# Experts of a mixture of experts: transposes in two groups among the products, and the weights' high parts on GpSimd

## The chip, the cores and the metric

The kernel runs on one core of one Trainium2 chip. The metric is the device time of one execution in microseconds. TensorE does the matrix products; VectorE, ScalarE and GpSimd work element by element; SyncE issues most of the transfers. The engines run their own instruction streams and meet only at semaphores.

## The reference

```python
def reference(q, k, v, proj, moe..., moe2...):
    x = attention(q, k, v, proj)            # 2 batches, 8 heads, 768 tokens, 64 wide: 1536 tokens x 512
    x = moe(x, ...)                         # what the change is about
    return mlp(x, w_in, w_out)              # 512 -> 2048 -> 512 with softplus

def moe(x, modality_id, w_gate, modality_bias, w1, w2):      # N 1536, D 512, E 8, F 1024
    logits = x @ w_gate + modality_bias[modality_id]
    e_idx = argmax(logits, axis=1)
    gate_w = softmax(logits)[arange(N), e_idx]
    for e in range(E):
        mask = e_idx == e
        h = maximum(x[mask] @ w1[e], 0.0)
        out[mask] = gate_w[mask, None] * (h @ w2[e])
    return out
```

Everything is in float32. Each token goes to one expert.

## The kernel before

It has three stages: attention, experts, and the last two layers (here MLP). Only the experts' stage is changed.

Tokens are sorted by expert on the chip, and each expert's tokens are worked through in tiles of 128. The number of tiles of an expert is data: every engine reads it from a table and runs one loop per expert, `Fori(0, n_e)`. `g` numbers the tiles through all experts. Tile 0 (part of the favourite expert) and tile 1 are done ahead by other code; the loops do tiles 2 on.

To keep float32 exactness on TensorE's faster fp32r path, each operand is split into a high part (the value rounded to fp32r) and a low part (value minus high part), and a product is made as high x high, low x high and high x low. So for each expert:

- SyncE loads `w1s[e % 2]` and `w2s[e % 2]` (2 MB each), once the expert that used the buffers is done.
- The high parts `w1h` (in two halves of 128x2048) and `w2h` (in four quarters of 128x1024) are copies by ScalarE (`w1_high`, `w2_high`). There is one `w1h` and one `w2h`, so the copy for expert e waits for `hB_done` (the last first-layer product of the expert before), or `y_done` (its last second-layer product).
- The low parts `w1l`, `w2l` are written in place of the loaded weights by VectorE (`w1_low`, `w2_low`, lines 1187 and 1194): loaded weight minus high part, both in SBUF.

And for each tile `g`, on TensorE, in this order:

- `w1_products`: 24 products of 512 columns into `psA[1]`, first half of the hidden features (12), then the second (12); each half in three parts of four: (`xth`, `w1h`), (`xtl`, `w1h`), (`xth`, `w1l`). They signal `hA_done` and `hB_done`.
- The rows of the hidden layer are copied by ScalarE from PSUM to `hrow` (`take_rows`), and TensorE transposes them: `turn_h(g, 0)`, `turn_y(g - 1)` (the previous tile's output rows) and `turn_h(g, 1)`, four 128x128 transposes each.
- ScalarE makes `hTh` from the transposed halves (`take_h`, with the Relu), and VectorE `hTl` (`low_h`, one input in PSUM, one in SBUF).
- `w2_products`: 24 products into `ps7`: for each half, eight with `hTh` (times `w2h`, `w2l`), then four with `hTl`. The last signals `y_done`.

Beside it ScalarE and VectorE make the next tile's `xth` (`high_x`) and `xtl` (`low_x`, both inputs in SBUF), and `x2h`, `x2l` for the MLP from the transposed output (`high_x2`, `low_x2`, PSUM and SBUF). Each engine works in program order: on VectorE `w1_low(e)` and `w2_low(e)` (six instructions) stand ahead of the loop over the expert's tiles, so ahead of its first `low_h`; before the loop of the last expert stand two `split_wi` as well. GpSimd's program goes from the gathering of the tokens' rows (line 595) to the MLP's `softplus`.

Of the kernel before, what the change touches and what calls it, by code (L numbers as in the profile page):

```python
# [10 lines left out]
ACT = mybir.ActivationFunctionType  # L11
# [17 lines left out]
DC = DM // P  # L29
E, F = 8, 1024  # L30
# [9 lines left out]
RING = 2  # L40
QUART = FC // 4
# [13 lines left out]
def build(nc, qk, v, proj, modality_id, fold_gate, modality_bias, w1, w2, w_in, w_out, out):  # L55
    ctx = ExitStack()
    with ctx:
# [249 lines left out]
        def loaded(e):  # L307

            return 16 * (e // RING + 1 + e % RING)
# [132 lines left out]
        def _(pool):  # L442
# [151 lines left out]
            for n in range(TILES):  # L594
                pool.indirect_dma_start(xin[:, n, :, :].rearrange("p h e -> p (h e)"), None, x_rows[:, :],
                                        bass.IndirectOffsetOnAxis(source[:, n:n + 1], 0)).then_inc(gathered[n], 16)

            def softplus(k, u):

                wait_reg(u_done, k + 1)  # L600
                pool.tensor_tensor(hres[u][:, :], hexp[u][:, :], hres[u][:, :], ALU.subtract).then_inc(c_done, 1)  # L601
                wait_reg(sum_done, k + 1)
                wait_reg(c_done, k + 1)
                pool.tensor_tensor(hsum[u][:, :], hsum[u][:, :], hres[u][:, :], ALU.add).then_inc(s_done, 1)  # L604
# [30 lines left out]
        def _(act):  # L635
# [85 lines left out]
            act.wait_ge(xT0_done, 1)  # L721
            nc.scalar.activation(xT0[:, :, :], psA[0][:, 1, :].rearrange("p (c n) -> p c n", c=DC), ACT.Copy).then_inc(xT0_ready, 1)

            def w1_high(e, first):

                act.wait_ge(w1_in[e % RING], loaded(e))
                if e:
                    act.wait_ge(hB_done, first)
                for h in range(2):
                    fs = slice(h * F // 2, (h + 1) * F // 2)  # L730
                    nc.scalar.activation(w1h[:, :, fs], w1s[e % RING][:, :, fs], ACT.Copy).then_inc(w1h_ready, 1)

            def w2_high(e, first):

                act.wait_ge(w2_in[e % RING], loaded(e))
                if e:
                    act.wait_ge(y_done, first)
                for h in range(4):
                    fs = slice(h * QUART, (h + 1) * QUART)
                    nc.scalar.activation(w2h[:, fs, :], w2s[e % RING][:, fs, :], ACT.Copy).then_inc(w2h_ready, 1)  # L740

            def gated(n):

# [6 lines left out]
            def high_x(g, at):  # L750

                act.wait_ge(hB_done, g)
                nc.scalar.activation(xth[:, :, :], xT[:, :, bass.ds(at, P)], ACT.Copy).then_inc(xh_ready, 1)

            def take_rows(g):

                for half, done, turned, ready in ((0, hA_done, tA_done, rA_ready), (1, hB_done, tB_done, rB_ready)):
                    act.wait_ge(done, g + 1)
                    act.wait_ge(turned, g - 1)
                    nc.scalar.activation(hrow[:, half * F // 2:(half + 1) * F // 2], psA[1][:, half, :], ACT.Copy).then_inc(ready, 1)  # L760

            def take_h(g, ps, doneA, doneB, count, halves=(0, 1)):

                for half in halves:
                    done, ready = ((doneA, hAh_ready), (doneB, hBh_ready))[half]
                    act.wait_ge(done, count)
                    nc.scalar.activation(hTh[:, half * FC // 2:(half + 1) * FC // 2, :],  # L767
                                         ps[:, half, :].rearrange("p (c n) -> p c n", c=FC // 2),
                                         ACT.Relu).then_inc(ready, 1)
# [25 lines left out]
                                     ACT.Copy).then_inc(woh_ready, 1)  # L795

            act.wait_ge(x_ready, PAIRS)
            w2_high(0, 0)
            act.wait_ge(lg_ready, 1)
            nc.scalar.activation(tmp8[:, :, :], tmp8[:, :, :], ACT.Exp).then_inc(gexp_done, 1)  # L800

# [4 lines left out]
                                     psA[1][:, half, :].rearrange("p (c n) -> p c n", c=FC // 2), ACT.Relu).then_inc(hT0_ready, 1)  # L806

            take_h0(0, hA_done)
            w1_high(0, 0)
            take_h0(1, hB_done)  # L810
            act.wait_ge(table_ready, 1)
            tiles_of = experts(act)
# [22 lines left out]
            high_x(2, nc.scalar.snap(nxt, min_val=0, max_val=B * S))  # L835
            for e in range(E):
                n_e, base_e, upto_e, first = next(tiles_of) if e else of_first
                if e:
                    w1_high(e, first)
                    w2_high(e, first)  # L840
                if e == E - 1:
                    for k in range(LAG):
                        split_wi(k, k)
                with nc.scalar.Fori(0 if e else 1, n_e) as i:
                    g = first + i
                    take_y(g - 1)
                    take_rows(g)
                    take_h(g, psA[2], tA_done, tB_done, g)
                    high_x2(g - 1, nc.scalar.snap(col, min_val=0, max_val=B * S))
                    act.reg_mov(col, nxt)  # L850
                    act.reg_mov(nxt, base_e + i * P + P)
                    act.reg_alu(nxt, nxt, upto_e, ALU.min)
                    high_x(g + 1, nc.scalar.snap(nxt, min_val=0, max_val=B * S))


            def softplus(k, u):
# [68 lines left out]
        def _(dve):  # L925
# [272 lines left out]
                dve.wait_ge(xT_done, n + 1)  # L1198
                V.tensor_copy(xT[:, :, n * P:(n + 1) * P], turn[n % 2].rearrange("p (c n) -> p c n", c=DC)).then_inc(xT_ready, 1)

            def low_h(g, ps):

                for half, high, ready in ((0, hAh_ready, hA_ready), (1, hBh_ready, hB_ready)):
                    fs = slice(half * FC // 2, (half + 1) * FC // 2)
                    dve.wait_ge(high, g)
                    V.scalar_tensor_tensor(hTl[:, fs, :], ps[:, half, :].rearrange("p (c n) -> p c n", c=FC // 2),  # L1206
                                           0.0, hTh[:, fs, :].bitcast(F32), ALU.max, ALU.subtract).then_inc(ready, 1)

            def low_x(g, at):

                dve.wait_ge(xh_ready, g - 1)
                V.tensor_tensor(xtl[:, :, :], xT[:, :, bass.ds(at, P)], xth[:, :, :].bitcast(F32), ALU.subtract).then_inc(xl_ready, 1)
# [42 lines left out]
            for e in range(E):  # L1255
                n_e, base_e, upto_e, first = next(tiles_of) if e else of_first
                if e:
                    w1_low(e)
                    w2_low(e)
                if e == E - 1:  # L1260
                    for k in range(LAG):
                        split_wi(k, k)
                with nc.vector.Fori(0 if e else 1, n_e) as i:
                    g = first + i
                    low_h(g, psA[2])
                    low_x2(g - 1, nc.vector.snap(col, min_val=0, max_val=B * S))
                    dve.reg_mov(col, nxt)
                    dve.reg_mov(nxt, base_e + i * P + P)
                    dve.reg_alu(nxt, nxt, upto_e, ALU.min)
                    low_x(g + 1, nc.vector.snap(nxt, min_val=0, max_val=B * S))  # L1270

            def softplus(k, u):
                dve.wait_ge(e_done, k + 1)
# [68 lines left out]
        def _(pe):  # L1342
            T = nc.tensor
# [203 lines left out]
                    last = turned(turn[n % 2][:, c * P:(c + 1) * P], xs_bits[n % 2][:, c * P:(c + 1) * P])  # L1547
                last.then_inc(xT_done, 1)

            def w1_products(e, g):  # L1550

                pe.wait_ge(xl_ready, g - 1)
                for half, done in ((0, hA_done), (1, hB_done)):
                    pe.wait_ge(w1h_ready, 2 * e + half + 1)
                    fs = slice(half * F // 2, (half + 1) * F // 2)
                    first = True
                    for x, w in ((xth, w1h), (xtl, w1h), (xth, w1l[e % RING])):
                        if w is not w1h:
                            pe.wait_ge(w1_split, 2 * e + half + 1)
                        for c in range(DC):  # L1560
                            last = T.matmul(psA[1][:, half, :], x[:, c, :], w[:, c, fs], start=first, stop=(w is not w1h and c == DC - 1))
                            first = False
                    last.then_inc(done, 1)

            def turn_h(g, half):

# [3 lines left out]
                    last = turned(psA[2][:, half, f * P:(f + 1) * P], hrow_bits[:, at:at + P])  # L1570
                last.then_inc((tA_done, tB_done)[half], 1)

            def w2_products(e, g):

                for half, high, low in ((0, hAh_ready, hA_ready), (1, hBh_ready, hB_ready)):
                    fs = range(half * FC // 2, (half + 1) * FC // 2)
                    pe.wait_ge(high, g)
                    for f in fs:
                        if f % QUART == 0:
                            pe.wait_ge(w2_split, 4 * e + f // QUART + 1)  # L1580
                        T.matmul(ps7[:, :], hTh[:, f, :], w2h[:, f, :], start=(f == 0), stop=False)  # L1581
                        T.matmul(ps7[:, :], hTh[:, f, :], w2l[e % RING][:, f, :], start=False, stop=False)
                    pe.wait_ge(low, g)
                    for f in fs:
                        last = T.matmul(ps7[:, :], hTl[:, f, :], w2h[:, f, :], start=False, stop=(f == FC - 1))
                last.then_inc(y_done, 1)
# [27 lines left out]
            for e in range(E):  # L1614
                n_e, _, _, first = next(tiles_of) if e else of_first
                with nc.tensor.Fori(0 if e else 1, n_e) as i:
                    g = first + i
                    w1_products(e, g)
                    turn_h(g, 0)
                    turn_y(g - 1)  # L1620
                    turn_h(g, 1)
                    w2_products(e, g)
            final = next(tiles_of)[3] - 1


# [117 lines left out]
```

## Time and profile before

| | us |
|---|---|
| median of 3 runs | 745.8 (745.42 to 746.28) |
| the profiled execution | 744.41 |
| its span in the trace | 742.6 |
| TensorE at work in the span | 719.3 (97%) |
| VectorE | 570.9 (77%) |
| ScalarE | 500.1 (67%) |
| GpSimd | 318.7 (43%) |

The experts' loops run from about 284 to 470 us of the span. In the profile PE is TensorE's products (PEld its weight loads, which overlap them), DVE VectorE, ACT ScalarE, POOL GpSimd, SP SyncE; a busy time is the time in which the engine had an instruction at work. Products are pipelined: one of 512 columns is shown with 0.39 us, but the next begins 0.2265 us after it.

### The profile page before, as it was taken

To read this page: it belongs to the slowest core of one execution; us is meant where nothing else is said; L and a number is where in the kernel's file an instruction comes from. 1 tells how busy PE (TensorE), PEld (TensorE's weight loads), DVE (VectorE), ACT (ScalarE), POOL (GpSimd) and SP (SyncE) were. 2 spreads that over 40 slices of the span, in tenths; PEclk is the share of its full clock that TensorE was granted. 3 is DMA by queue.
4 is the path that set the end of the run, shared out by engine and by line. 5 is a ranking of instruction groups with operands and counts; after the bars stand their busy time and mean duration, and the time that the engine had idled before them with its cause. 6 is when DMAs were issued, how large, how long until landed. Compare 5 with 4: busy or idle time off the path is not lost. (4 is left out here: it accounts for less than half of the span.)

```text
span 742.6 us, 13137 instructions
## 1 busy us (share of the span) xinstructions
PE 719.3 (97%) x4017; PEld 607.1 (82%) x4017; DVE 570.9 (77%) x944; ACT 500.1 (67%) x916; POOL 318.7 (43%) x289
## 2 busy tenths in 40 slices
PE   5999999999999999999999999999999999999996
PEld 4888888989988778888888878778887888878884
DVE  6999999999999666449992181598788787887874
ACT  6888788888887654559993372565656656566562
POOL 7777566778741450000000000155554755557543
PEclk9999999999999999999999999999999999999999
DMA  3811111104133268328991000032322423225221
GB/s 128 291 49 44 53 38 46 59 18 161 40 109 137 100 195 333 117 113 315 353 357 51 0 29 0 30 113 85 113 86 85 167 87 110 90 86 169 85 85 57
DMA packets 40531, 85.05 MB, mean 115 GB/s; under 512 B 5584, under 2 KB 9840, under 8 KB 40496
## 3 DMA queue, kind: packets, MB, share of 16 engines
q1 hardware_dynamic: 37776, 77.01, 30.4%
q0 software_dynamic: 2000, 6.98, 2.8%
q10 hardware_dynamic: 720, 0.64, 0.2%
q8 instruction: 17, 0.28, 0.2%
q14 instruction: 18, 0.15, 0.1%
HBM read 76.82 MB, written 6.68 MB: 112 GB/s over the span
## 5 line engine op out<-in xcount | busy, mean ns | idle before, releaser
L601 POOL TENSOR_TENSOR hres<-hexp,hres 128x512 f32<-128x512 f32 x46 | 59.7, 1298 | 303.7 <-DVE hres L1274 303.6
L668 ACT ACTIVATE pTh<-psA 128x384 fp32r<-128x384 f32 x192 | 83.9, 491 | 38.2 <-PE psA L1382 37.8
L949 DVE TENSOR_TENSOR pTl<-psA,pTh 128x384 fp32r<-128x384 f32 x192 | 97.7, 551 | 8.8 <-ACT pTh L668 7.9
L1376 PE MATMUL psA<-K,Q 128*128 128x384 f32 x384 | 92.5, 364 | 3.3 <-ACT K L705 2.1
L942 DVE TENSOR_SCALAR_CACHE_REDUCE psA<-psA 128x768 f32<-128x768 f32 x96 | 91.8, 956 | 3.2 <-PE psA L1376 3.1
L659 ACT ACTIVATE probs<-psA,negmax 128x768 f32<-128x768 f32 x96 | 87.4, 910 | 2.9 <-DVE psA L942 2.5
L1222 DVE TENSOR_TENSOR wil<-rawi,wih 128x512 fp32r<-128x512 f32 x48 | 79.1, 1650 | 6.6 <-ACT wih L787 6.6
L859 ACT ACTIVATE habs<-psA 128x512 f32<-128x512 f32 x48 | 28.6, 597 | 76.8 <-PE psA L1638 76.8
L1206 DVE SCALAR_TENSOR_TENSOR hTl<-psA,hTh 128x512 fp32r<-128x512 f32 x32 | 21.4, 688 | 73.1 <-ACT hTh L767 72.8
L1382 PEld LDWEIGHTS psA<-ident_r,probs_bits 128*128 128x128 f32 x576 | 59.3, 143 | 17.3 <-issue 6.8
L604 POOL TENSOR_TENSOR hsum<-hsum,hres 128x512 f32<-128x512 f32 x46 | 69.6, 1514 | 8.2 <-POOL hres L601 8.2
L1652 PE MATMUL psA<-woh,sh 128*128 128x512 f32 x184 | 72.1, 392 | 0.7 <-DVE sl L1291 0.7
L1382 PE MATMUL psA<-ident_r,probs_bits 128*128 128x128 f32 x576 | 70.8, 252 | 1.3 <-DVE pTl L949 0.7
L1653 PE MATMUL psA<-wol,sh 128*128 128x512 f32 x184 | 71.6, 389 | 0.0
L1654 PE MATMUL psA<-woh,sl 128*128 128x512 f32 x184 | 71.6, 389 | 0.0
L1376 PEld LDWEIGHTS psA<-K,Q 128*128 128x128 f32 x384 | 64.2, 193 | 6.1 <-issue 4.9
L1405 PE MATMUL ps<-pTh,vhl 128*128 128x384 f32 x186 | 62.8, 338 | 0.1
L1405 PE MATMUL ps<-pTl,vhl 128*128 128x384 f32 x186 | 62.5, 336 | 0.0
L1291 DVE TENSOR_TENSOR sl<-hsum,sh 128x512 fp32r<-128x512 f32 x47 | 53.6, 1140 | 1.8 <-ACT sh L873 1.8
L1638 PE MATMUL psA<-x2h,wih 128*128 128x512 f32 x192 | 51.7, 391 | 0.8 <-DVE hsum L1282 0.7
L1581 PE MATMUL ps<-w2h,hTh 128*128 128x512 f32 x128 | 51.6, 403 | 0.0
L1638 PE MATMUL psA<-x2l,wih 128*128 128x512 f32 x192 | 51.4, 389 | 0.0
(243 smaller groups left out, 1656.1 us busy)
## 6 DMA issues: line engine op xcount, KB each, us to landing
w2s<-in_moe_w SPq DMA_DIRECT2D x9, 2048.0 KB, 9.4
w1s<-in_moe_w SPq DMA_DIRECT2D x9, 2048.0 KB, 9.1
rawi<-in_moe_w_in SPq DMA_DIRECT2D x48, 256.0 KB, 2.6
rawo<-in_moe_w_out SPq DMA_DIRECT2D x48, 256.0 KB, 2.8
raw<-in_qk SPq DMA_DIRECT2D x16, 384.0 KB, 3.1
vs<-in_v SPq DMA_DIRECT2D x16, 192.0 KB, 2.4
x_rows<-X SPq DMA_DIRECT2D x1, 1728.0 KB, 6.8
x_rows<-X SPq DMA_DIRECT2D x1, 1512.0 KB, 5.5
```

The lines of the kernel that those rows point to most:

```text
L659: nc.scalar.activation(probs[u % 2][:, :].rearrange("p (a n) -> p a n", a=2), psA[u % 2][:, :, 0:HALF], ACT.Exp, bias=negmax[:, u % 4:u % ...
L668: nc.scalar.activation(pTh[u // TPGR % 2][:, g * TPH:(g + 1) * TPH, u % TPGR * P:(u % TPGR + 1) * P], psA[2][:, g, 0:HALF].rearrange("p (t ...
L942: V.tensor_scalar(psA[u % 2][:, :, 0:HALF], psA[u % 2][:, :, 0:HALF], PENALTY, PENALTY, ALU.min, ALU.min, accum_out=negmax[:, u % 4:u % 4 ...
L949: V.tensor_tensor(pTl[u // TPGR % 2][:, g * TPH:(g + 1) * TPH, cols], psA[2][:, g, 0:HALF].rearrange("p (t n) -> p t n", t=TPH), pTh[u // ...
L1222: V.tensor_tensor(wil[u][:, :, :], rawi[u][:, :, :], wih[u][:, :, :].bitcast(F32), ALU.subtract).then_inc(wi_split, 1)
L1376: last = T.matmul(psA[u % 2][:, h, 0:HALF], qs[par][:, cols], ks[par][:, h * HALF:(h + 1) * HALF], start=start, stop=not start)
L1382: return T.transpose(out.bitcast(F32R), rows_bits, ident_r[:, :])
L1405: last = T.matmul(last_ps if type(G) is int and G == PAIRS - 1 else ps6[:, 0:COLS], vhl[gm // 2 % 2][:, kt, :], p[gm % 2][:, kt, :], start ...
L1638: last = T.matmul(hps[u], w[u][:, d, :], x[:, d, g * GTOK:(g + 1) * GTOK], start=first, stop=(w is wil and d == DC - 1))
L1652: T.matmul(acc[t], sh[u][:, cols], woh[u][:, :], start=first, stop=False)
L1653: T.matmul(acc[t], sh[u][:, cols], wol[u][:, :], start=False, stop=False)
L1654: last = T.matmul(acc[t], sl[u][:, cols], woh[u][:, :], start=False, stop=final)
```

## The change

On TensorE the two groups of transposes of hidden rows are moved apart. The tile's order becomes: the twelve products of the first half; parts 0 and 1 of the second half; `turn_h(g, 0)` and `turn_y(g - 1)`; part 2 of the second half; the eight high products of the first half of the second layer; `turn_h(g, 1)`; the rest. ScalarE and VectorE order their per-half work to match. And for experts 1 to 7 the copies that make `w1h` and `w2h` go from ScalarE to GpSimd, which in this stage had nothing to do; expert 0's stay on ScalarE. `wait_reg` is GpSimd's wait on a semaphore followed by an increment of another.

```diff
+            pool.wait_ge(table_ready, 1)
+            tiles_of = experts(pool)
+            next(tiles_of)
+            for e in range(1, E):
+                _, _, _, first = next(tiles_of)
+                wait_reg(w1_in[e % RING], loaded(e))
+                wait_reg(hB_done, first)
+                for h in range(2):
+                    fs = slice(h * F // 2, (h + 1) * F // 2)
+                    pool.tensor_copy(w1h[:, :, fs], w1s[e % RING][:, :, fs]).then_inc(w1h_ready, 1)
+                    wait_reg(w1h_ready, 2 * e + h + 1)
+                wait_reg(w2_in[e % RING], loaded(e))
+                wait_reg(y_done, first)
+                for h in range(4):
+                    fs = slice(h * QUART, (h + 1) * QUART)
+                    pool.tensor_copy(w2h[:, fs, :], w2s[e % RING][:, fs, :]).then_inc(w2h_ready, 1)
+                    wait_reg(w2h_ready, 4 * e + h + 1)
...
             for e in range(E):
                 n_e, base_e, upto_e, first = next(tiles_of) if e else of_first
-                if e:
-                    w1_high(e, first)
-                    w2_high(e, first)
...
                 with nc.scalar.Fori(0 if e else 1, n_e) as i:
                     g = first + i
                     take_y(g - 1)
-                    take_rows(g)
-                    take_h(g, psA[2], tA_done, tB_done, g)
+                    take_rows(g, 0)
+                    take_h(g, psA[2], tA_done, tB_done, g, (0,))
                     high_x2(g - 1, nc.scalar.snap(col, min_val=0, max_val=B * S))
...
+                    take_rows(g, 1)
                     high_x(g + 1, nc.scalar.snap(nxt, min_val=0, max_val=B * S))
+                    take_h(g, psA[2], tA_done, tB_done, g, (1,))
...
-                    low_h(g, psA[2])
+                    low_h(g, psA[2], (0,))
                     low_x2(g - 1, nc.vector.snap(col, min_val=0, max_val=B * S))
...
                     low_x(g + 1, nc.vector.snap(nxt, min_val=0, max_val=B * S))
+                    low_h(g, psA[2], (1,))
...
+            def w1_products(e, g, half, parts):
+
+                done = (hA_done, hB_done)[half]
+                fs = slice(half * F // 2, (half + 1) * F // 2)
+                for part in parts:
+                    x, w = ((xth, w1h), (xtl, w1h), (xth, w1l[e % RING]))[part]
...
@@ w2_products
                         T.matmul(ps7[:, :], hTh[:, f, :], w2l[e % RING][:, f, :], start=False, stop=False)
+                    if half == 0 and turning:
+                        turn_h(g, 1)
                     pe.wait_ge(low, g)
...
                     g = first + i
-                    w1_products(e, g)
+                    pe.wait_ge(xl_ready, g - 1)
+                    w1_products(e, g, 0, (0, 1, 2))
+                    w1_products(e, g, 1, (0, 1))
                     turn_h(g, 0)
                     turn_y(g - 1)
-                    turn_h(g, 1)
-                    w2_products(e, g)
+                    w1_products(e, g, 1, (2,))
+                    w2_products(e, g, turning=True)
```

## Rows read from the trace of the kernel before

**Rows 1.** Windows of two tiles: us, busy of PE, PEld, DVE, ACT, POOL, PEclk, DMA, GB/s

```profile
309.00:321.40 12.40, 12.35 (x62) 10.16 (x61) 2.59 (x4) 3.90 (x7) 0.00 (x0) 1.00 0.00 0
...
370.86:383.21 12.35, 12.29 (x61) 10.12 (x60) 11.44 (x11) 11.18 (x13) 0.00 (x0) 1.00 0.91 336
```

**Rows 2.** Timeline of ScalarE, experts' stage: start us, us, what

```profile
296.98 3.91 ACT L740 ACTIVATE w2h<-w2s 128x1024 fp32r<-128x1024 f32 x4 [0.52 <-PE ps L1585]
...
329.80 3.72 ACT L731 ACTIVATE w1h<-w1s 128x2048 fp32r<-128x2048 f32 x2
334.05 3.91 ACT L740 ACTIVATE w2h<-w2s 128x1024 fp32r<-128x1024 f32 x4 [0.54 <-PE ps L1585]
...
383.47 3.91 ACT L740 ACTIVATE w2h<-w2s 128x1024 fp32r<-128x1024 f32 x4 [0.52 <-PE ps L1585]
...
432.91 3.91 ACT L740 ACTIVATE w2h<-w2s 128x1024 fp32r<-128x1024 f32 x4 [0.53 <-PE ps L1585]
```

**Rows 3.** Waits of 285 to 472 us: total us, times, longest

```profile
PEld psA L1382 <- ACT hrow L760: 3.8, 15, 1.0
```

**Rows 4.** Timeline of one tile's turn from first to second layer

```profile
375.40 1.07 PE L1561 MATMUL psA<-w1l,xth 128*128 128x512 f32 x4
...
376.31 0.45 PE L1382 MATMUL psA<-ident_r,hrow_bits 128*128 128x128 f32 x4
...
376.51 0.60 ACT L760 ACTIVATE hrow<-psA 128x512 f32<-128x512 f32 x1 [0.51 <-PE psA L1561]
...
377.16 0.40 PEld L1382 LDWEIGHTS psA<-ident_r,hrow_bits 128*128 128x128 f32 x4 [0.20 <-ACT hrow L760]
...
377.65 0.50 PE L1581 MATMUL ps<-w2h,hTh 128*128 128x512 f32 x1
```

**Rows 5.** Timeline of TensorE where the MLP begins

```profile
471.28 1.07 PE L1638 MATMUL psA<-x2l,wih 128*128 128x512 f32 x4
472.19 1.07 PE L1638 MATMUL psA<-x2h,wil 128*128 128x512 f32 x4
473.10 0.46 PE L1382 MATMUL ps<-ident_r,yrow_bits 128*128 128x128 f32 x4
...
474.40 1.08 PE L1638 MATMUL psA<-x2l,wih 128*128 128x512 f32 x4
```

**Rows 6.** GpSimd's casts, groups by form: busy us, mean ns, idle before

```profile
L515 POOL CAST vhl<-vs 128x384 fp32r<-128x384 f32 x16 | 8.0, 503 | 50.0 <-PE ps L1405 50.0
...
L464 POOL CAST ident_r<-ident 128x128 fp32r<-128x128 f32 x1 | 0.3, 288 | 0.0
```

**Rows 7.** Timeline of VectorE, boundary to expert 7

```profile
429.01 0.68 DVE L1212 TENSOR_TENSOR xtl<-xT,xth 128x512 fp32r<-128x512 f32 x1
430.61 4.50 DVE L1187 TENSOR_TENSOR w1l<-w1s,w1h 128x2048 fp32r<-128x2048 f32 x2 [0.92 <-ACT w1h L731]
435.02 4.62 DVE L1194 TENSOR_TENSOR w2l<-w2s,w2h 128x1024 fp32r<-128x1024 f32 x4
...
439.56 1.29 DVE L1222 TENSOR_TENSOR wil<-rawi,wih 128x512 fp32r<-128x512 f32 x2
```

**Rows 8.** Timeline of GpSimd and VectorE, three places where they meet

```profile
500.72 1.52 POOL L604 TENSOR_TENSOR hsum<-hsum,hres 128x512 f32<-128x512 f32 x1 [0.18 <-POOL hres L601]
501.01 1.78 DVE L1222 TENSOR_TENSOR wil<-rawi,wih 128x512 fp32r<-128x512 f32 x1
...
212.17 0.83 POOL L497 CAST Q<-qs 64x768 fp32r<-64x768 f32 x1
...
212.55 0.48 DVE L1032 TENSOR_SCALAR chosen<-chosen,code 128x8 f32<-128x8 f32 x1
...
6.62 0.95 DVE L1099 TENSOR_TENSOR K<-raw,K 64x768 fp32r<-64x768 f32 x1
6.87 0.91 POOL L488 CAST K<-bits 12x192 fp32r<-12x192 f32 x1 [0.44 <-DVE bits L1097]
```

**Rows 9.** VectorE's PSUM-reading subtraction: duration ns min/median/max, first, last start

```profile
L949 DVE TENSOR_TENSOR pTl<-psA,pTh x192: 540/548/560, 15.5 to 243.8; 128x384 fp32r<-128x384 f32 x192
```

**Rows 10.** Granted clock in 40 slices, and TensorE's longest wait (total, times, longest)

```profile
PEclk9999999999999999999999999999999999999999
...
PE ps L1353 <- ACT hashc L695: 4.5, 1, 4.5
```

More of the change, by code:

```diff
@@ L722, in _, with w1_high_first, w2_high_first @@
             nc.scalar.activation(xT0[:, :, :], psA[0][:, 1, :].rearrange("p (c n) -> p c n", c=DC), ACT.Copy).then_inc(xT0_ready, 1)
-            def w1_high(e, first):
-                act.wait_ge(w1_in[e % RING], loaded(e))
-                if e:
-                    act.wait_ge(hB_done, first)
+            def w1_high_first():
+                act.wait_ge(w1_in[0], loaded(0))
                 for h in range(2):
                     fs = slice(h * F // 2, (h + 1) * F // 2)
[L731 to L737, printed above, removed]
+                    nc.scalar.activation(w1h[:, :, fs], w1s[0][:, :, fs], ACT.Copy).then_inc(w1h_ready, 1)
+            def w2_high_first():
+                act.wait_ge(w2_in[0], loaded(0))
                 for h in range(4):
                     fs = slice(h * QUART, (h + 1) * QUART)
-                    nc.scalar.activation(w2h[:, fs, :], w2s[e % RING][:, fs, :], ACT.Copy).then_inc(w2h_ready, 1)
+                    nc.scalar.activation(w2h[:, fs, :], w2s[0][:, fs, :], ACT.Copy).then_inc(w2h_ready, 1)
             def gated(n):
@@ L753, in high_x, with take_rows @@
                 nc.scalar.activation(xth[:, :, :], xT[:, :, bass.ds(at, P)], ACT.Copy).then_inc(xh_ready, 1)
[L755 to L760, printed above, removed]
+            def take_rows(g, half):
+                done, turned, ready = ((hA_done, tA_done, rA_ready), (hB_done, tB_done, rB_ready))[half]
+                act.wait_ge(done, g + 1)
+                act.wait_ge(turned, g - 1)
+                nc.scalar.activation(hrow[:, half * F // 2:(half + 1) * F // 2], psA[1][:, half, :], ACT.Copy).then_inc(ready, 1)
             def take_h(g, ps, doneA, doneB, count, halves=(0, 1)):
@@ L797, in _ @@
             act.wait_ge(x_ready, PAIRS)
-            w2_high(0, 0)
+            w2_high_first()
             act.wait_ge(lg_ready, 1)
@@ L808, in _ @@
             take_h0(0, hA_done)
-            w1_high(0, 0)
+            w1_high_first()
             take_h0(1, hB_done)
@@ L837, in _ @@
                 n_e, base_e, upto_e, first = next(tiles_of) if e else of_first
-                if e:
-                    w1_high(e, first)
-                    w2_high(e, first)
                 if e == E - 1:
@@ L1199, in take_xT, with low_h @@
                 V.tensor_copy(xT[:, :, n * P:(n + 1) * P], turn[n % 2].rearrange("p (c n) -> p c n", c=DC)).then_inc(xT_ready, 1)
-            def low_h(g, ps):
-                for half, high, ready in ((0, hAh_ready, hA_ready), (1, hBh_ready, hB_ready)):
+            def low_h(g, ps, halves=(0, 1)):
+                for half in halves:
+                    high, ready = ((hAh_ready, hA_ready), (hBh_ready, hB_ready))[half]
                     fs = slice(half * FC // 2, (half + 1) * FC // 2)
@@ L1548, in turn_x @@
                 last.then_inc(xT_done, 1)
[L1550 to L1563, printed above, removed]
+            def w1_products(e, g, half, parts):
[3 more added lines that the diff above has]
+                    x, w = ((xth, w1h), (xtl, w1h), (xth, w1l[e % RING]))[part]
+                    if part == 0:
+                        pe.wait_ge(w1h_ready, 2 * e + half + 1)
+                    elif part == 2:
+                        pe.wait_ge(w1_split, 2 * e + half + 1)
+                    for c in range(DC):
+                        last = T.matmul(psA[1][:, half, :], x[:, c, :], w[:, c, fs], start=(part == 0 and c == 0),
+                                        stop=(part == 2 and c == DC - 1))
+                    if part == 2:
+                        last.then_inc(done, 1)
             def turn_h(g, half):
@@ L1571, in turn_h, with w2_products @@
                 last.then_inc((tA_done, tB_done)[half], 1)
-            def w2_products(e, g):
+            def w2_products(e, g, turning=False):
                 for half, high, low in ((0, hAh_ready, hA_ready), (1, hBh_ready, hB_ready)):
```

## The prediction

> **What bounds the kernel now.** I read the windows of single tiles first. In the experts' stage a tile of 128 tokens takes 12.35 to 12.4 us with TensorE at work for all but some 0.05 us of it, whether it is a middle tile of a long expert (VectorE at work 2.59 us) or a one-tile expert (VectorE 11.44, ScalarE 11.18, GpSimd 0.00) [rows 1]. So TensorE sets the pace of all 15 looped tiles, but in one-tile experts VectorE and ScalarE have under 1 us of slack each. The starts of w2's high parts on ScalarE give the layout: expert 0 ends at 296.98; 37.07 us (three tiles) later expert 1 ends at 334.05; from there to 383.47 four boundaries lie 12.35 us apart, so experts 2 to 5 have one tile each; expert 6 has four tiles (to 432.91) and expert 7 the last three [rows 2]. GpSimd does nothing in the stage.
>
> Then the waits. In the stage TensorE's weight loads wait for ScalarE's copy of the second half of the hidden rows: 3.8 us in 15 waits, 0.25 a tile [rows 3]. In the timeline of one tile the twelve transposes begin at 376.31, are held 0.20 us before the last four until the copy that started at 376.51 ends, and the second-layer products begin at 377.65 [rows 4].
>
> **What the change saves.** 48 products 512 wide at 0.2265 us (0.907 for four, from 471.28 to 472.19 and on) are 10.87 us; the tile's other 1.48 us are the twelve transposes with their wait and switches. Four transposes alone between products, nothing waited for, cost this: from 472.19 to 474.40 are eight products (1.81) and one such group, 0.40 us [rows 5]. Three fours are 1.2 us. With the third part of the second half's products and then the high products of the first half between copy and transpose, neither copy is waited for: 0.28 us less a tile, 12.07 us, for 15 tiles -4.2 us. Lower bound of the gain: 0, if the extra switch between transposes and products eats it; no row shows the new order. take_rows, take_h, low_h are only reordered; their 0.6 and 0.69 us stay off the path, since first-half rows still have products and transposes between them and their use.
>
> **What GpSimd's copies cost alone.** For each of experts 1 to 7, two copies of 128x2048 and four of 128x1024. GpSimd's casts take 0.288 us for 128 elements and 0.503 for 384, so 0.18 + 0.00084 n: 1.89 us and 1.04 us [rows 6]. That is what ScalarE takes (3.72 for two, 3.91 for four [rows 2]), 8 us of GpSimd in a 12.35 us tile. Taken alone it fits, and ScalarE is relieved of 7.6 us an expert; but ScalarE wasn't on the path, so this relief earns nothing beyond the 4.2.
>
> **What they cost together with VectorE.** The low parts are VectorE subtractions with both inputs in SBUF: two in 4.50 us, four in 4.62, and low_x 0.68 [rows 7]. The trace shows what happens when GpSimd works in SBUF at the same time. VectorE's 128x512 subtraction, 0.68 us alone [rows 7], took 1.78 from 501.01, to 502.79: 0.55 after GpSimd's instruction ended at 502.24. An instruction of only 8 elements a partition took 0.48 and ended at 213.03, with GpSimd's cast of 212.17 ending at 213.00. The other way, a cast of only 12x192 took 0.91 us and ended at 7.78, 0.21 after VectorE's two-input subtraction ended at 7.57 [rows 8]. So whoever comes second waits for the whole instruction, and that holds for casts too. Where VectorE reads one input from PSUM nothing is lost: 192 such subtractions beside GpSimd's work stay between 540 and 560 ns [rows 9]; hTl and x2l are of that kind.
>
> The Trainium skill ("SBUF — State Buffer", Who interferes with whom) says the same as a rule: a VectorE instruction with two SBUF inputs and a GpSimd one that reads SBUF share a port pair under an exclusive lock, and the second to issue fully blocks. By it no part of a copy would overlap a subtraction, as in my sum; the rows above agree for instructions under 1.8 us, and no row shows 2 us casts. Without it (rows for short ones not carrying over) the sum would be -4.2 alone.
>
> Pure passes, start-up excluded (GpSimd 0.836 n ns; VectorE n/0.96 ns, of whose 0.68 us for 512 that leaves 0.15 of start-up): copies 2x1.71 + 4x0.86 = 6.8; subtractions 2x2.13 + 4x1.07 + 0.53 = 9.1; together 15.9 us of the shared resource per expert. With every start-up counted it is 17.7. A one-tile expert offers 12.07.
>
> **The queue at a boundary**, 0 being hB_done of the previous expert's last tile. GpSimd wakes at some 0.18 (its gap at 500.72 [rows 8]): first half of w1h to 2.1; low_x behind it to 2.6; second half to 4.3; hTl's second half (needs no port) 3.7; w1l first to 6.4; then alternately (y_done is at 5.8, so GpSimd now queues too) w2h quarter 0 to 7.3, w1l second 9.4, quarter 1 10.3, w2l 0 11.4, quarter 2 12.2, w2l 1 13.3, quarter 3 14.1, w2l 2 15.2, w2l 3 16.3, and only then, VectorE being in order, hTl's first half of the new tile, 17.0. TensorE begins the new tile at 5.7, finds both halves of w1 in time (needed at 5.7 and 8.4; low ones 7.5 and 11.0), reaches the second layer at 11.9, waits 0.6 for w2l 1, transposes to 14.6 and waits 2.4 for hTl. Loss: 3.0 us, at experts 1 and 6. At experts 2 to 5 the next expert's w1 copy (its hB_done was at 11.9) is already queued behind quarter 3 and gets in ahead of w2l 3: 1.7 more, 4.7; the tile is 16.8, not far over the 15.9 of passes. At expert 7 VectorE has two w_in splits as well before hTl (1.29 us for two [rows 7]): 4.2.
>
> Sum: 4x4.7 + 2x3.0 + 4.2 = 29.0, less 4.2: **+24.8 us**. Profiled execution 744.4 (its span 742.6 and 1.8 around): 769.2. The median of the runs, 745.8, is 1.4 above that execution: 770.6, forecast **770.5**.
>
> Bounds. Below: only part of each copy excludes VectorE, half the loss: 29.0/2 - 4.2 = +10, 756. Above: every hand-over is paid in full with start-up and semaphore: two times (1.89 + 0.18 + 2.28 + 0.05), four times (1.04 + 0.18 + 1.22 + 0.05), low_x 0.68 (0.05 as from ScalarE's end at 377.11 to 377.16 [rows 4]): 19.4 us, so +7.4 over 12.07 four times; at the other boundaries some 1.5 of the 2.6 that this adds to 16.8 lies ahead of hTl, so 4.5 twice and 5.7 once; less 4.2: +40, 786. I take the alternation since the rows show a blocked instruction ending 0.55 after its release, a pass without start-up.
>
> **Rivals.**
> 1. Faster: the exclusion doesn't carry over to long casts (or is brief at their start), so the copies hide in idle GpSimd. Place: w1l and w2l; price 0; it decides if copy and subtraction overlap so far that the per-expert chain is under 12.07 us instead of 15.9. Then -4.2: 741.6. For it: GpSimd idle all stage, ScalarE near full. Against: three kinds of collisions in the trace. 5 in 100.
> 2. Half the loss, 756, by partial overlap or a luckier order of grants. 11 in 100.
> 3. Paid in full, 786: VectorE or GpSimd keeps coming too late for a grant. 10 in 100.
> 4. TensorE's clock falls in the new stalls of about 4 us. In every slice it is granted in full now, and the longest wait, 4.5 us, stands ahead of the first products [rows 10], so the trace says neither. Price: the 16 products left of the second layer (3.6 us) at 1.2 instead of 2.4 GHz take 3.6 more, at five boundaries up to 18: 788. 9 in 100. The Trainium skill ("TensorE: Matmul & The Clock Gate", summary table) advises against idle gaps between bursts for this reason; no run here shows it.
> 5. The change doesn't do what it says in its order part: transposes still wait, gain 0, 774. Within the forecast's range.
>
> The forecast with 5 has 65 in 100; likely range 764 to 776. The range for 8 in 10 reaches from 2 to 3: 756 to 786. About 0.2% (1.5 us) is what can be told from no change. Faster 0.06 (rival 1 and a bit of 2), same 0.02, slower 0.92.
>
> **What would show it.** VectorE's w1l subtractions up from 2.28 us to about 4 and w2l from 1.22 to about 2 where casts run; GpSimd casts also lengthened above 1.89 and 1.04; a wait of TensorE for hTl at each boundary's first low products, 2.4 us at experts 1 and 6 and 4 at 2 to 5; tiles without a boundary at 12.07 with no wait for hrow. Wrong if casts and subtractions keep their lengths side by side, if the tile of experts 2 to 5 stays near 12.1, or if the granted clock falls below full after the stalls.

## The result

Before 745.51 us (six runs, 744.98 to 746.28), after 776.24 us (six runs, 775.08 to 779.65): ratio 1.0411, 95% interval 1.0397 to 1.0426, 30.7 us slower. The forecast was 770.5, range 756 to 786. The profiled execution of the changed kernel has a span of 773.3 us against 742.6, 30.7 more.

All but 0.4 us of it lies in the experts' loops. In the changed kernel the first copy of output rows after tile 1 starts at 284.99 and the last at 501.28, 216.3 us for 15 tiles; between the same copies of the kernel before it is 186.0 (284.56 to 470.58, ScalarE's line 774). The page of the kernel after: share of busy time of each engine, then of the 40 slices the rows of TensorE and of its clock.

```profile
PE 728.8 (94%) x4017; PEld 612.7 (79%) x4017; DVE 600.9 (78%) x944; ACT 450.5 (58%) x874; POOL 405.4 (52%) x331
...
PE   5999999999999998997798997999999999999996
...
PEclk9999999999999999998999999999999999999998
```

Windows of single tiles, which answer to [rows 1]: first tile of expert 1, a middle tile of it, then experts 2, 3, 4 and 5 (one tile each), first tiles of 6 and 7. Columns as there; the last but two is the granted clock.

```profile
296.81:313.71 16.90, 14.04 (x61) 11.12 (x60) 13.34 (x10) 4.00 (x7) 7.90 (x4) 0.90 0.43 154
313.71:325.78 12.07, 12.07 (x62) 9.96 (x60) 2.69 (x4) 4.00 (x7) 0.00 (x0) 1.00 0.00 0
337.82:357.16 19.34, 14.82 (x61) 11.67 (x60) 19.34 (x12) 4.00 (x7) 12.88 (x6) 0.82 0.66 241
357.16:370.79 13.63, 12.24 (x61) 10.05 (x60) 9.89 (x10) 4.01 (x7) 11.79 (x6) 1.00 0.84 309
370.79:391.20 20.41, 15.32 (x61) 11.63 (x60) 20.41 (x12) 4.00 (x7) 13.86 (x6) 0.83 0.56 207
391.20:404.74 13.54, 12.25 (x61) 10.05 (x60) 9.80 (x10) 4.01 (x7) 11.69 (x6) 1.00 0.90 329
404.74:422.66 17.92, 14.52 (x61) 10.99 (x60) 14.29 (x10) 4.00 (x7) 8.84 (x4) 0.90 0.45 162
458.84:476.96 18.12, 14.10 (x61) 11.10 (x60) 14.52 (x12) 4.00 (x7) 7.87 (x4) 0.91 0.09 29
```

The middle tile takes 12.07 us as forecast, ScalarE is at work for 4 us in any tile, and the seven first tiles of experts 1 to 7 take 119.9 us where the kernel before needed 87.2 (six of 12.34 to 12.38, and 13.01 at expert 7, where TensorE waited 0.62 us for hrow). VectorE is at work without a gap in experts 2 and 4, and in three of the rows shown the clock's mean is 0.90 or 0.91, in two 0.82 and 0.83. (The kernel before had 1.00 in both [rows 1].)

The waits of TensorE in the stage (total, times, longest; PE's rows, as the wait of the weight load before it repeats the same time) show who held it:

```profile
PE ps L1603 <- DVE hTl L1220: 18.4, 7, 3.9
...
PE ps L1597 <- DVE w2l L1207: 4.2, 7, 0.7
```

The wait for hrow of [rows 3] is gone. The groups of casts and subtractions in the stage (busy us, mean ns | idle before):

```profile
L613 POOL CAST w2h<-w2s 128x1024 fp32r<-128x1024 f32 x28 | 55.5, 1982 | 20.6 <-PE ps L1603 17.1 <-POOL w2h L613 3.5
...
L1207 DVE TENSOR_TENSOR w2l<-w2s,w2h 128x1024 fp32r<-128x1024 f32 x28 | 48.9, 1788 | 7.5 <-POOL w2h L613 7.5
L1200 DVE TENSOR_TENSOR w1l<-w1s,w1h 128x2048 fp32r<-128x2048 f32 x16 | 44.7, 2834 | 0.0
...
L607 POOL CAST w1h<-w1s 128x2048 fp32r<-128x2048 f32 x14 | 31.5, 2248 | 85.5 <-PE psA L1576 82.4 <-POOL w2h L613 1.9 <-POOL w1h L607 1.2
```

Alone a cast of 1024 takes 1.05 us and one of 2048 1.90 (their shortest in this trace, at 391.54 and 332.29); the means are 1.98 and 2.25. The w2l subtraction goes from 1.22 us (mean in the kernel before; four in 4.62 in [rows 7]) to 1.79, the w1l subtraction from 2.29 to 2.83.

And this is what follows the waits. Timeline of TensorE, the first four products with hTl after each wait, experts 1 to 4:

```profile
308.40 2.08 PE L1603 MATMUL ps<-w2h,hTl 128*128 128x512 f32 x4 [2.22 <-DVE hTl L1220]
...
351.09 2.08 PE L1603 MATMUL ps<-w2h,hTl 128*128 128x512 f32 x4 [3.92 <-DVE hTl L1220]
...
367.03 1.20 PE L1603 MATMUL ps<-w2h,hTl 128*128 128x512 f32 x4 [1.39 <-DVE hTl L1220]
...
385.04 2.08 PE L1603 MATMUL ps<-w2h,hTl 128*128 128x512 f32 x4 [3.92 <-DVE hTl L1220]
```

Four such products take 1.07 us at the full clock. After the waits shown of 2.22 and 3.92 us they take 2.08, the lower level, 1.2 GHz: in the window 308.40 to 311.80 the granted clock is 0.52, in 351.00 to 354.50 it is 0.50. The moment of the fall differs: at expert 2 it lies within the wait (1.00 until 349.20, 0.52 in the next us, the wait ends at 351.09), at expert 7 only after the wait of 3.42 us (1.00 until 472.00, the wait ended at 471.61, 0.56 in the next us). After the wait of 1.39 us they take 1.20, as after any restart. From the end of the wait to the next tile's first product there are 16 products: 3.76 us at expert 3, but 5.31, 6.07, 6.16, 5.37 and 5.35 us at experts 1, 2, 4, 6 and 7 (waits of 2.22, 3.92, 3.92, 2.22 and 3.42 us). The sum over 3.76 is **9.5 us** that the lower clock costs.

### The profile page after: what moved, and what is told of

Same layout as the page of the kernel before. It is cut to its first block and busy times, and to the rows that moved or that the text cites. A ratio compares the mean times of both kernels' runs of the same rounds, so it can differ in the third digit from the quotient of the medians.

```text
span 773.3 us, 13225 instructions
## 1 busy us (share of the span) xinstructions
PE 728.8 (94%) x4017; PEld 612.7 (79%) x4017; DVE 600.9 (78%) x944; ACT 450.5 (58%) x874; POOL 405.4 (52%) x331
## 5 line engine op out<-in xcount | busy, mean ns | idle before, releaser
L607 POOL CAST w1h<-w1s 128x2048 fp32r<-128x2048 f32 x14 | 31.5, 2248 | 85.5 <-PE psA L1576 82.4
L613 POOL CAST w2h<-w2s 128x1024 fp32r<-128x1024 f32 x28 | 55.5, 1982 | 20.6 <-PE ps L1603 17.1
L1207 DVE TENSOR_TENSOR w2l<-w2s,w2h 128x1024 fp32r<-128x1024 f32 x32 | 53.7, 1717 | 7.5 <-POOL w2h L613 7.5
L1597 PE MATMUL ps<-w2h,hTh 128*128 128x512 f32 x128 | 54.6, 427 | 4.2 <-DVE w2l L1207 4.2
```

## The experiments

The experiments ran on two chips on which the kernel before takes 752.7 and 752.6 us instead of 745.5; so ratios and differences to it are compared.

**The order alone.** GpSimd's block is left out, and ScalarE has the copies again:

```diff
                 n_e, base_e, upto_e, first = next(tiles_of) if e else of_first
+                if e:
+                    w1_high(e, first)
+                    w2_high(e, first)
```

> The new order of products and transposes alone; all high parts stay on ScalarE. Account of the prediction (ScalarE is not on the path, the order gains 0.28 us in each of 15 tiles): 745.5 - 4.2 = 741.3 us. Rival: on ScalarE the second half of hTh now comes after the second layer has begun, so at a boundary the six copies of weights start later and end later, and the copy of the next tile's first rows, queued behind them, is late for transposes that the new order wants eight products earlier: about 1.2 us of wait for hrow at each of 7 boundaries, the tiles without a boundary still at 12.06. That gives 745.5 + 7 x 0.9 - 8 x 0.29 = about 749.5 us.

Measured: ratio 1.0039 (1.0025 to 1.0052), 2.8 us slower (755.49 against 752.69). The rival was right, in kind and in size (4 us were expected). Timeline of the first tile of expert 1:

```profile
305.85 3.89 ACT L740 ACTIVATE w2h<-w2s 128x1024 fp32r<-128x1024 f32 x4
...
309.64 0.58 ACT L774 ACTIVATE yrow<-ps 128x512 f32<-128x512 f32 x1
310.12 0.59 ACT L760 ACTIVATE hrow<-psA 128x512 f32<-128x512 f32 x1
310.76 0.54 PE L1386 MATMUL psA<-ident_r,hrow_bits 128*128 128x128 f32 x4 [0.77 <-ACT hrow L760]
```

TensorE waits 0.77 us for rows that ScalarE copies only after the four quarters of w2h, and the boundary tiles of experts 1 to 6 take 13.07 us, that of expert 7, after a wait of 1.82, 14.10; tiles without a boundary take 12.05. So the order's gain of 0.28 us a tile is real in eight tiles and is lost in seven. In the changed kernel it is had everywhere only because ScalarE has been relieved.

**GpSimd's copies alone.** The kernel before, with the new block on GpSimd and without `w1_high`, `w2_high` in the loop on ScalarE:

```diff
                 n_e, base_e, upto_e, first = next(tiles_of) if e else of_first
-                if e:
-                    w1_high(e, first)
-                    w2_high(e, first)
```

> The old order of products and transposes, with the high parts of experts 1 to 7 on GpSimd. If the loss is the collision of casts and subtractions alone, it is all here, plus the 4.2 us that the order gives back: 745.5 + 30.7 + 4 = about 780 us, and tiles without a boundary stay at 12.35. If the new order has a part in the loss (the second half of hTl, made late, stands ahead of w1's low parts on VectorE), it is clearly less: 770 us or under.

Measured: 1.0424 (1.0405 to 1.0444), 31.0 us slower (783.66). The loss is here without the new order. 35 were expected, the 30.7 and the order's gain. The tiles without a boundary are at 12.36 to 12.40, so they lose some 2.5 us against the changed kernel; but the seven first tiles take 117.3 us, 2.6 less than there. In them TensorE waits 0.4 us for w2l instead of 4.2, and about as long for hTl:

```profile
PE ps L1600 <- DVE hTl L1221: 19.4, 7, 4.2
```

The clock falls at four of the seven boundaries here, not at five. Experts 1 and 2 wait nearly the same time, and only at expert 2 does the clock fall (timeline of TensorE):

```profile
314.94 1.21 PE L1600 MATMUL ps<-w2h,hTl 128*128 128x512 f32 x4 [2.75 <-DVE hTl L1221]
...
355.09 2.07 PE L1600 MATMUL ps<-w2h,hTl 128*128 128x512 f32 x4 [2.69 <-DVE hTl L1221]
```

The granted clock is 1.00 from 312.10 to 318.94, through the first wait and all products after it, and 0.50 from 355.09 to 358.00.

**GpSimd writes, but doesn't read.**

```diff
-                    pool.tensor_copy(w1h[:, :, fs], w1s[e % RING][:, :, fs]).then_inc(w1h_ready, 1)
+                    pool.memset(w1h[:, :, fs].bitcast(F32), 0.0).then_inc(w1h_ready, 1)
...
-                    pool.tensor_copy(w2h[:, fs, :], w2s[e % RING][:, fs, :]).then_inc(w2h_ready, 1)
+                    pool.memset(w2h[:, fs, :].bitcast(F32), 0.0).then_inc(w2h_ready, 1)
```

> As the changed kernel, but GpSimd fills w1h and w2h with zeros instead of copying the weights into them (so the products with the high parts of experts 1 to 7 are left out of the result): as many elements written, nothing read from SBUF. If the loss comes of GpSimd and VectorE both reading SBUF, it goes away and only the gain of the order is left: 741.3 us, subtractions back at 2.28 and 1.22 us, every tile at 12.06. If GpSimd's mere activity or its place in the chain of semaphores is the cause, it stays within 10 us of 776.

Measured: 0.9947 (0.9933 to 0.9960), 3.8 us faster (748.89 against 752.69). Groups by form in the stage:

```profile
L1200 DVE TENSOR_TENSOR w1l<-w1s,w1h 128x2048 fp32r<-128x2048 f32 x16 | 35.9, 2282 | 0.0
...
L613 POOL MEMSET w2h<- 128x1024 f32 x28 | 26.8, 958 | 17.9 <-PE ps L1603 14.7 <-POOL w2h L613 3.2
L607 POOL MEMSET w1h<- 128x2048 f32 x14 | 25.4, 1815 | 97.4 <-PE psA L1576 96.3 <-POOL w1h L607 1.1
```

Fills nearly as long as the casts alone, in the same chain of semaphores, and the subtractions are back at 2.28 us; the tiles of the stage, boundaries too, take 12.06 us but for expert 7's first, 12.38. So neither GpSimd's activity nor its place in the chain costs anything: what costs is that it reads SBUF. That VectorE must read it with both inputs shows in the changed kernel, where three VectorE instructions of 512 columns, 0.68 us each when alone, fall beside one cast (timelines of GpSimd and VectorE):

```profile
349.52 2.66 POOL L607 CAST w1h<-w1s 128x2048 fp32r<-128x2048 f32 x1 [0.17 <-POOL w1h L607]
...
350.35 0.68 DVE L1220 SCALAR_TENSOR_TENSOR hTl<-psA,hTh 128x512 fp32r<-128x512 f32 x1
350.95 0.68 DVE L1231 TENSOR_TENSOR x2l<-ps,x2h 128x512 f32 x1
351.55 1.17 DVE L1226 TENSOR_TENSOR xtl<-xT,xth 128x512 fp32r<-128x512 f32 x1
```

The two with an input in PSUM keep their 0.68 us; the one with both inputs in SBUF takes 1.17 and ends 0.54 after the cast. This run is also what the order is worth when nothing else stands in its way: forecast 4.2, measured 3.8.

**VectorE writes, but doesn't read, for w2.** The casts as in the changed kernel, and on VectorE:

```diff
+                    if e:
+                        V.memset(w2l[e % RING][:, fs, :].bitcast(F32), 0.0).then_inc(w2_split, 1)
+                        continue
                     V.tensor_tensor(w2l[e % RING][:, fs, :], w2s[e % RING][:, fs, :],
```

> As the changed kernel, but VectorE fills w2's low parts of experts 1 to 7 with zeros instead of subtracting (the products with them are left as products with zeros): same elements written, nothing read. The casts stay as they are. If only instructions of both engines that read SBUF exclude each other, the shared passes of a one-tile expert are 6.8 + 4.8 = 11.6 us, under the tile's 12.06: no wait for hTl over 0.5 us, GpSimd's w2h casts back near 1.04 us, clock full, total 0 to 4 us faster than before. If VectorE's writing is enough to exclude GpSimd, the loss stays above 20 us.

Measured: 1.0040 (1.0030 to 1.0051), 2.6 us slower (755.18 against 752.6). Timeline of one tile:

```profile
377.81 6.43 DVE L1200 TENSOR_TENSOR w1l<-w1s,w1h 128x2048 fp32r<-128x2048 f32 x2
...
382.26 2.88 POOL L613 CAST w2h<-w2s 128x1024 fp32r<-128x1024 f32 x1 [0.17 <-POOL w2h L613]
...
385.31 1.04 POOL L613 CAST w2h<-w2s 128x1024 fp32r<-128x1024 f32 x1 [0.17 <-POOL w2h L613]
385.47 0.91 DVE L1208 MEMSET w2l<- 128x1024 f32 x1 [0.16 <-issue]
386.52 1.04 POOL L613 CAST w2h<-w2s 128x1024 fp32r<-128x1024 f32 x1 [0.17 <-POOL w2h L613]
```

Beside VectorE's fills casts take 1.04 us; beside its w1l subtraction one takes 2.88 and the two subtractions 6.43 instead of 4.50. The mechanism is confirmed from the other side: VectorE's writing doesn't exclude GpSimd. The total was expected 0 to 4 us faster and is 2.6 slower: with 11.6 us of passes in a tile of 12.06, TensorE still waits for hTl, 0.94 us in a one-tile expert and 1.68 at expert 7, where at most 0.5 was expected. The sum of passes isn't the whole condition; the chain from y_done through two casts held by w1l to hTl has its own length: the last fill of w2l waits for the last cast, which ends at 387.56, and hTl starts at 388.67, right behind that fill.

**Only w1's copies on GpSimd**, w2's on ScalarE as before (the block on GpSimd ends after the two w1h casts; ScalarE's loop has `w2_high(e, first)`).

> New order; only w1's high parts on GpSimd, w2's back on ScalarE. The shared passes of a one-tile expert are 3.4 (casts) + 9.1 (subtractions) = 12.5 us, just over the tile's 12.06, instead of 15.9. Theory (the loss goes by how far the sum of passes exceeds the tile): waits for hTl under 1 us, no fall of the clock, some 0.7 us of wait for hrow at each boundary since ScalarE still makes w2's high parts ahead of the rows: 0 to 4 us slower than before. Rival (each collision costs by itself, six collisions of an expert becoming two): a third of the loss, 10 us slower.

Measured: 1.0018 (1.0007 to 1.0029), 1.4 us slower. No wait for hTl is left among TensorE's waits; what there is, is for hrow (4.5 us in 7 waits), as in the order-only run. Two of six casts, half of the elements, cost TensorE nothing by their collisions (w1l's mean is 2.70 us, so they do collide), where six cost over 30 us: the loss isn't per collision, but begins when the queue of casts and subtractions outgrows the time to hTl. Nor does the sum of passes alone tell where: it was 12.5 us here, without a wait for hTl, and 11.6 in the run before, with one.

**A filler for the waits.**

```diff
                     if half == 0 and turning:
                         turn_h(g, 1)
+                        for f in range(12):
+                            T.matmul(psA[0][:, f % 2, :], hTh[:, f % 4, :], w2h[:, f % 4, :], start=True, stop=True)
```

> As the changed kernel, with 12 needless products (512 columns, 2.7 us, into a buffer that the stage does not use) in every tile ahead of the wait for the low parts of the hidden layer. Where TensorE now waits they fall into the wait; in the other 8 tiles and where the wait is short they cost up to 2.7 us. Theory that the waits bring the clock down and that this costs some 10.5 us: four products after the wait take 1.07 us and not 2.08, and the total is 776.2 + 8 x 2.7 + 3 - 10.5 = about 790 us. Rival, the products after the wait are slow for another reason (the hTl or weights coming late one by one): they stay slow, total about 801 us.

Measured: 1.0574 (1.0558 to 1.0591), 42.7 us slower (795.41); expected were 44.5 over the kernel before (790 against 745.5). The waits for hTl that remain are 1.1 us, and the products after them run at the full clock:

```profile
379.19 1.20 PE L1605 MATMUL ps<-w2h,hTl 128*128 128x512 f32 x4 [1.09 <-DVE hTl L1220]
...
396.10 1.19 PE L1605 MATMUL ps<-w2h,hTl 128*128 128x512 f32 x4 [1.11 <-DVE hTl L1220]
```

The window of the stage has a granted clock of 1.00 (in the changed kernel, 284 to 502 us, 0.95):

```profile
284.00:500.00 216.00, 210.69 (x1032) 172.77 (x1031) 134.64 (x109) 59.73 (x106) 83.81 (x42) 1.00 0.38 135
```

The seven first tiles take 110.4 us here, 9.4 less than in the changed kernel, though each has 2.7 us more work; experts 3, 4 and 5, where the shared resource sets the pace, take 16.8 to 16.9 us each. It is a test by cost and not a cure: the other eight tiles go from 12.06 to 14.78.

**A version that uses what was learned.** All high parts on ScalarE, and the second group of transposes (with the output's) after four instead of eight high products; on ScalarE the rows are copied ahead of `take_y`, and `high_x` ahead of the second half of hTh (VectorE's order to match):

```diff
-                    take_y(g - 1)
                     take_rows(g, 0)
+                    take_y(g - 1)
                     take_h(g, psA[2], tA_done, tB_done, g, (0,))
-                    high_x2(g - 1, nc.scalar.snap(col, min_val=0, max_val=B * S))
                     take_rows(g, 1)
...
                     high_x(g + 1, nc.scalar.snap(nxt, min_val=0, max_val=B * S))
                     take_h(g, psA[2], tA_done, tB_done, g, (1,))
+                    high_x2(g - 1, nc.scalar.snap(act_x2, min_val=0, max_val=B * S))
...
+                        if f == 1 and turning:
+                            turn_h(g, 1)
+                            turn_y(g - 1)
```

> All high parts on ScalarE as in the kernel before, and an order made for that: ScalarE copies the first rows ahead of the output rows; the second group of transposes, with the output's, stands after four instead of eight high products of the second layer; high_x goes ahead of the second half of hTh. So the six weight copies begin about 0.6 us earlier after a boundary than in the order-only run and the rows are copied 0.5 us earlier in the queue: wait for hrow at a boundary 0.1 to 0.4 us instead of 1.0, tiles without a boundary 12.06. Then 8 x -0.29 and 7 x (-0.2 to +0.1), +0.9 at the last expert: 1 to 3 us faster than before (0.2 to 0.4%). Rival: the queue of ScalarE at a boundary is the limit whatever the order (some 11.9 us of work in 12.06): no gain or a loss of 1 to 3 us.

Measured: 0.9963 (0.9950 to 0.9976), 3.1 us faster than the kernel before (749.5 against 752.6). The first tiles of experts 1 to 6 take 12.25 to 12.29 us, the other tiles 12.01 to 12.06, and the first tile of expert 7, with the two w_in splits ahead of its rows, about 13.3 (25.4 from 429.05 to 454.42 for it and its neighbour). The rival is out. It is the only version with the reference's full arithmetic that beats both kernels.

## Why the prediction was right, and where its sizes were off

**Direction and place** were right: the loss lies in the casts and subtractions at expert boundaries, and TensorE feels it as a wait for hTl and a smaller one for w2l. The three experiments that take reading away (0.9947), move it all (1.0424) or move two copies of six (1.0018) show it. But one of the prediction's own signs of being wrong came true as well, the granted clock below full after the waits, and the total came as near as it did partly by luck: by the terms below, waits and the order's gain made the sum 7.3 us too high, and the clock and the restarts, left out, made it 12.8 too low.

**The mutual exclusion** carried over from instructions under 1.8 us to casts of 1.9 us, by rows and experiments. The sign given for it was too large: w1l subtractions were forecast at about 4 us and have a mean of 2.83, w2l at about 2 and have 1.79. The Trainium skill's rule ("SBUF — State Buffer", Who interferes with whom) held in the detail that was not tested ahead: a GpSimd instruction that only writes SBUF doesn't contend with VectorE's two-input ones, nor GpSimd with a VectorE instruction that has at most one SBUF input, outside VectorE's 2-port modes. Here subtractions took 2.28 us beside GpSimd's fills, and casts 1.04 beside VectorE's.

**The gain of the order** was forecast 0.28 us a tile; tiles without a boundary take 12.02 to 12.07 us, down from 12.35 to 12.4, with no wait for hrow. What the prediction passed over is that this needs ScalarE relieved: "this relief earns nothing beyond the 4.2" is true of the old order only. With the new order and no relief the kernel is 2.8 us slower. It also passed over the first tile of expert 7, which takes 13.01 us in the kernel before and not 12.35.

**The queue at a boundary.** Forecast were tiles of 15.1 (experts 1 and 6), 16.8 (2 to 5) and 16.3 (7), 113.5 us; measured 119.9. Waits were forecast at 29.0 us in total and are 22.6. At expert 1 the forecast was 0.6 for w2l and 2.4 for hTl; the trace has 0.64 and 2.22. For 2 to 5 it was 4.7 each. They alternate instead: 4.5 and 1.4, 5.1 and 1.3. While TensorE waits long and is then slow, GpSimd and VectorE finish the next expert's w1 parts (expert 3's w1l subtractions end at 357.73, and its tile begins at 357.16), and the next boundary starts with these out of the way. This fits the times, but no run tests it by itself. In the filler run, with no fall of the clock and 2.7 us more work in a tile, the alternation is gone: 16.9 us for experts 4 and 5, where 16.8 was worked out.

**The term that was missing** is the clock. It stood as rival 4 with 9 in 100 and a price of up to 18 us; it happens at five of seven boundaries and costs 9.5 us. The price of 3.6 us a boundary took all 16 products as slow; the clock came back before the last of them, so it was 1.6 to 2.4. The prediction could say that no run shows such a fall; now two kernels do. Put beside the waits: 22.6 + 9.5 + some 3 for restarts after 14 waits is what the seven first tiles take over 12.06 each, 35.4 us. The gain in all 15 tiles, 186.0 less 15 x 12.06, is 5.1 (0.7 of it the wait for hrow at expert 7); that leaves 30.3 us, the stage's own difference. The forecast's sum is 24.8, low by 5.5: waits too high by 6.4, the gain too low by 0.9, clock and restarts left out with 12.8. So the total was nearer than its terms. The claim that the trace of before "says neither" was fair; that four waits of about 4 us deserved more than 9 in 100 can be said only with hindsight.

**Not settled**: which waits bring the clock down. In the changed kernel it stayed full after 1.39 us and less and fell after 2.22 us and more. But the length alone doesn't decide: with the copies alone on GpSimd it stayed full after 2.75 us and fell after 2.69. Waits of 1.82 us (the order alone) and 1.68 us (fills for w2l) left it full.

## What to carry to other kernels

An idle engine isn't free for a job if, as here, both it and a neighbour that works with two SBUF inputs read SBUF in the same period: sum the time in which GpSimd reads SBUF and that in which VectorE works with two SBUF inputs over the shortest period, and compare it with the period (here 15.9 against 12.06), then follow the chain to the instruction that the bound engine awaits: 11.6 us of passes still made it wait, and 12.5 in another arrangement did not. Price a wait of TensorE with what the clock takes after it, not only with its length. And an engine with slack on average can be the limit of a new order: here ScalarE's queue at a boundary decided whether moving transposes gave 3 us or cost 3.

## What the runs showed of the hardware

- The clock fell to 1.2 GHz with a wait of TensorE of 2.22 us, and the products ran at it until 311.8, 3.4 us; with a wait of 3.92 us until about 355.9, 4.9 us. With equal waits it fell once (2.69 us) and stayed full once (2.75 us).
- GpSimd and VectorE don't disturb each other if either only writes SBUF: casts of 1.04 us beside fills of 0.91, subtractions of 2.28 us beside fills of 1.81.
- An instruction that is held takes up to the whole of its neighbour's on top: casts of 128x1024 took 2.88 us, 1.84 over their own 1.04, while the w1l subtraction of 2.28 us ran.
